# Expert units of 384 or 448 rows, with a transposed second product

## The reference

```
# layer A: every row goes to one expert
expert_idx = argmax(xn @ en.T / tau);  gate_w = softmax(...)[expert_idx]
for e in range(8):
    h = maximum(x[mask] @ w1[e], 0);  out[mask] = gate_w * (h @ w2[e])
# layer B, on layer A's rows: rows with x @ w_skip > 0 alone are computed
e_idx = argmax(x @ w_gate);  gate_w = softmax(...)[e_idx]
out = x + gate_w * (maximum(x @ w1[e], 0) @ w2[e])     # other rows: out = x
```

## Time and profile before

| | us |
|---|---|
| median of 3 runs | 739.09 |
| the profiled execution | 744.15 |
| its span, first to last instruction | 742.4 |
| TensorE matmul busy | 676.3 (91%) |
| VectorE busy | 440.2 (59%) |
| ScalarE busy | 316.8 (43%) |
| GpSimd busy | 170.1 (23%) |
| mean granted TensorE clock | 0.954 |

### The profile page before, as it was taken

How to read it: one execution, slowest core, us unless ns; L and a number is a source line. 1 busy time by engine, 2 the same in 40 slices (tenths; PEclk the granted TensorE clock), 3 DMA queues, 4 the chain that set the end, 5 groups by cost and what they waited for, 6 DMA issues and landing times.

```text
span 742.4 us, 16385 instructions
## 1 busy us (share of the span) xinstructions
PE 676.3 (91%) x5328; PEld 649.5 (87%) x5329; DVE 440.2 (59%) x987; ACT 316.8 (43%) x548; POOL 170.1 (23%) x195
## 2 busy tenths in 40 slices
PE   5999999999879999999899999997699999998992
PEld 4999899998769999989889999997699999998892
DVE  5787978978527455573555655643356564555630
ACT  3565666755215435342534444431253443535520
POOL 4221233252430030321233203123210110111111
PEclk9899999999589999999999999998599999999997
DMA  9688998790145526340701552500266724645400
GB/s 155 86 139 141 172 188 147 98 189 19 64 142 203 174 86 213 119 167 17 254 20 51 206 199 72 167 29 23 80 230 215 253 83 178 231 147 196 140 1 23
DMA packets 142882, 98.65 MB, mean 133 GB/s; under 512 B 106431, under 2 KB 133738, under 8 KB 142816
## 3 DMA queue, kind: packets, MB, share of 16 engines
q1 hardware_dynamic: 135520, 85.14, 44.6%
q0 software_dynamic: 7296, 12.73, 4.9%
HBM read 78.77 MB, written 28.89 MB: 145 GB/s over the span
## 4 chain that ended last, share of the span: by engine, by line
PE 74%; DVE 9%; issue 9%; ACT 3%; DMA 2%; SPq 1%; DVEq 1%; POOL 0%; ACTq 0%; POOLq 0%
PE bank_a L922 6%; PE banks_y L798 6%; PE bank_a L924 6%; PE bank_a L923 6%; PE banks_y L932 5%; PE banks_y L934 5%; PE banks_y L933 5%; PE banks_s L777 3%; DVE w_lo L1313 3%; PE bank_a L853 3%; PE bank_b L934 2%; PE bank_b L932 2%; PE bank_b L933 2%; PE banks_y L790 2%; PE bank_b L922 2%
## 5 line engine op out<-in xcount | busy, mean ns | idle before, releaser
L1313 DVE TENSOR_TENSOR w_lo<-raw_w,w_hi 128x768 fp32r<-128x768 f32 x128 | 116.6, 953 | 8.6 <-DVE kept L1664 3.6
L922 PE MATMUL bank_a<-x_hi,w_hi 128*128 128x384 f32 (+1 forms) x342 | 109.6, 321 | 5.8 <-DVE w_lo L1313 3.1
L924 PE MATMUL bank_a<-x_hi,w_lo 128*128 128x384 f32 (+1 forms) x342 | 106.8, 312 | 0.0
L923 PE MATMUL bank_a<-x_lo,w_hi 128*128 128x384 f32 (+1 forms) x342 | 106.8, 312 | 0.0
L1195 ACT ACTIVATE h_hi<-bank_a 128x384 fp32r<-128x384 f32 (+1 forms) x114 | 50.2, 440 | 122.9 <-PE bank_a L924 122.8
L1063 ACT ACTIVATE w_hi<-raw_w 128x768 fp32r<-128x768 f32 x128 | 99.2, 839 | 0.0
L636 POOL DMA_INDIRECT sorted_rows<-row_send,slot_idx x33 | 36.0, 1090 | 232.2 <-DVE slot_idx L1586 225.5
L1620 DVE SCALAR_TENSOR_TENSOR h_lo<-bank_a,h_hi 128x384 fp32r<-128x384 f32 (+1 forms) x114 | 55.8, 493 | 50.6 <-ACT h_hi L1195 47.8
L932 PE MATMUL banks_y<-w_hi,h_hi 128*128 128x384 f32 x232 | 79.8, 344 | 2.1 <-DVE row_out L1602 1.2
L934 PE MATMUL banks_y<-w_hi,h_lo 128*128 128x384 f32 x232 | 78.1, 337 | 0.0
L933 PE MATMUL banks_y<-w_lo,h_hi 128*128 128x384 f32 x232 | 78.0, 336 | 0.0
(11 more groups left out here) (216 smaller groups left out, 1399.5 us busy)
## 6 DMA issues: line engine op xcount, KB each, us to landing
raw_w<-in_moe_w SPq DMA_DIRECT2D x30, 1536.0 KB, 7.0
sorted_rows<-pad_row SPq DMA_DIRECT2D x16, 388.0 KB
raw_f<-in_f_logit SPq DMA_DIRECT2D x32, 144.0 KB, 4.3
raw_k<-in_k SPq DMA_DIRECT2D x32, 144.0 KB, 4.3
raw_q<-in_q SPq DMA_DIRECT2D x32, 144.0 KB, 4.9
raw_v<-in_v SPq DMA_DIRECT2D x32, 144.0 KB, 3.1
xs<-sorted_rows SPq DMA_DIRECT2D x22, 194.0 KB, 4.3
xs<-sorted_rows SPq DMA_DIRECT2D x10, 388.0 KB, 5.0
```

What stands on the lines that cost most here:

```text
L922: pe.matmul(bank, hi, x_hi[:, kd, cols], start=(kd == 0), stop=False)
L923: pe.matmul(bank, hi, x_lo[:, kd, cols], start=False, stop=False)
L924: ins = pe.matmul(bank, lo, x_hi[:, kd, cols], start=False, stop=(kd == KD - 1))
L1313: dve.tensor_tensor(w_lo[par][:, sl, :], raw_w[:, sl, :], w_hi[par][:, sl, :].bitcast(F32), ALU.subtract).then_inc(w_split_lo, 1)
```

## The change

Layer A gets code of its own. Its plan (`plan_mixed`) counts an expert's rows in blocks of 64 and makes units of 448 rows (`LARGE`) or 384 rows (`SMALL`): up to 6 blocks are one small unit, 7 blocks one large unit, more are large units and at most one small one. The second product is transposed as well: w2 stationary, the unit's hidden values moving, 24 matmuls for each of three blocks of 128 output columns. ScalarE copies its result, `y_t`, and both the logits and the rows are made from it in the next unit: `route_logits` uses `y_t` as it is, `turn_rows` turns it back with 12 transposes, and VectorE scales each tile straight into `row_send`. The next unit's rows are loaded, turned and split within the second product. There are four slots of rows for a unit, the fourth with 64 rows. Layer B keeps the old units; it waits for four slots to be sent, and `row_out` is now the same memory as `row_send`.

```diff
-    REG = N + 2 * P
+    REG = N + 3 * P
+    MIXED_SLOTS = 4
+    SMALL, LARGE = 3 * P, 3 * P + HB
+        y_t = sb("y_t", [P, KD, LARGE])
...
+        def over_mixed(engine, unit):
+            engine.wait_ge(plan_ready[0], 1)
+            with engine.Fori(0, E // 2) as e2:
+                for par in range(2):
...
+                    with engine.If(small > 0):
+                        unit(par, e, u0, SMALL, 0, small)
+                    with engine.If(larges > 0):
+                        with engine.Fori(0, larges) as j:
+                            unit(par, e, u0 + small + j, LARGE, j, small)
...
# SP
+                        sp.wait_ge(f["kept"], u + 1)
+                        load_mixed(size, e * REG + j * LARGE + small * (0 if size == SMALL else SMALL))
+                        def next_expert():
+                            with sp.If(e < E - 1):
+                                pad(within(e + 1, 1, E - 1))
...
+                            wait_split(sp, e, 1)
+                            load_next(0, e, par, load_w1)
+                            wait_split(sp, e, 2)
+                            load_next(0, e, par, load_w2)
...
# TensorE
+                def take_mixed(next_u, s=s):
+                    pe.wait_ge(s["xs_first"], 16 * (next_u + 1))
+                    pe.wait_ge(s["xs_second"], 16 * (next_u + 1))
+                    for kd in range(KD):
+                        for slot in range(SLOTS):
+                            pe.transpose(ps_take[kd][:, slot * P:(slot + 1) * P], xs[0][:, slot, kd * P:(kd + 1) * P], ident[:])
+                        pe.transpose(ps_take[kd][:, SMALL:LARGE], xs_more[:, kd * P:(kd + 1) * P],
+                                     ident[0:HB, 0:HB]).then_inc(s["xt"], 1)
+                def contract_mixed(par, size, kd, kf):
+                    bank = ps_yt[kd][:, 0:size]
+                    hi, lo = (w2_slice(w[par][:], kf)[:, kd * P:(kd + 1) * P] for w in (w_hi, w_lo))
+                    pe.matmul(bank, hi, h_hi[:, kf, 0:size], start=(kf == 0), stop=False)
+                    pe.matmul(bank, hi, h_lo[:, kf, 0:size], start=False, stop=False)
+                    return pe.matmul(bank, lo, h_hi[:, kf, 0:size], start=False, stop=(kf == KF - 1))
+                def unit_mixed(par, e, u, size, j, small, s=s):
+                    wait_split(pe, e, 1)
+                    pe.wait_ge(s["x_lo"], KD * u + KD)
+                    for kf in range(KF):
+                        if kf >= 3:
+                            pe.wait_ge(s["h_lo"], KF * u + kf - 2)
+                        expand_mixed(par, size, kf)
+                        if kf == 0:
+                            route_logits(u)
+                        if kf == 1:
+                            turn_rows(u)
+                        if kf == 4:
+                            rank(g, u + 1, MIXED_SLOTS, ps_rank_u, ps_count_u)
+                    wait_split(pe, e, 2)
+                    pe.wait_ge(s["row"], MIXED_SLOTS * u + 7)
+                    for kd in range(KD):
+                        if kd == 2:
+                            pe.wait_ge(s["y_copied"], KD * u + KD + 1)
+                        for kf in range(KF):
+                            if kd == 0:
+                                pe.wait_ge(s["h_lo"], KF * u + kf + 1)
+                            ins = contract_mixed(par, size, kd, kf)
+                            if kd == 1 and kf == 2:
+                                take_mixed(u + 1)
+                        ins.then_inc(s["y"], 1)
...
+                def route_logits(u, s=s):
+                    pe.wait_ge(s["y_copied"], KD * u + KD)
+                    pe.wait_ge(g["slot"], u + 1)
+                    for slot in range(MIXED_SLOTS):
+                        n = slot_rows(slot)
+                        for kd in range(KD):
+                            ins = pe.matmul(ps_logit_u[0:n, slot, 0:E + 1], y_t[:, kd, slot * P:slot * P + n], gate_w_t[:, kd, :],
...
+                def turn_rows(u, s=s):
+                    pe.wait_ge(s["row"], MIXED_SLOTS * u + 3)
...
+                            ins = pe.transpose(ps_row[slot][0:n, kd * P:(kd + 1) * P], y_t[:, kd, slot * P:slot * P + n], ident[:])
+                        ins.then_inc(s["turned"], 1)
...
# ScalarE, unit_mixed
+                    for kf in range(KF):
+                        act.wait_ge(s["h"], KF * u + kf + 1)
+                        act.activation(h_hi[:, kf, 0:size], ps_h[kf % 3][:, 0:size], ACT.Relu).then_inc(s["h_hi"], 1)
+                        if kf == 4:
+                            softmax(g, u, MIXED_SLOTS)
+                    in_first_mixed(act, size, j, small, lambda: split_four(e + 1, 1 - par, w1_in, 0))
+                    copy_y(size, u, 0)
+                    x_high_mixed(u + 1)
...
+                    in_first_mixed(act, size, j, small, second_weights)
+                    copy_y(size, u, 1)
+                    copy_y(size, u, 2)
...
# VectorE, unit_mixed, behind the low part of each block kf
+                        if kf == 1:
+                            pick_rows(ch, u)
+                        if kf == 3:
+                            rows_to_send((0, 1), u)
+                        if kf == 4:
+                            rows_to_send((2, 3), u)
+                            keep_mixed(ch, size, u)
+                        if kf == 6:
+                            place_rows(ch, u)
+                    in_first_mixed(dve, size, j, small, lambda: split_four(e + 1, 1 - par, 0))
+                    x_low_mixed(u + 1)
...
+                    in_first_mixed(dve, size, j, small, second_weights)
...
+            def rows_to_send(slots, u):
...
+                    dve.wait_ge(s["turned"], MIXED_SLOTS * u + slot + 1)
+                    dve.tensor_scalar(row_send[0:n, slot, 0:DM], ps_row[slot][0:n, :], kept[0:n, slot, 0:1], None,
+                                      ALU.mult).then_inc(s["row"], 1)
...
+            def keep_mixed(ch, size, u):
...
+                dve.wait_ge(s["row"], MIXED_SLOTS * u + 7)
+                ch.link(dve.tensor_copy(kept[:, 0:SLOTS, :], xs[0][:, :, GATE:GATE + 2]))
...
+                dve.tensor_copy(kept[0:HB, SLOTS, :], more).then_inc(s["kept"], 1)
...
# pick_rows
-                ch.link(dve.tensor_reduce(mx, ps_logit_u[:, :, 0:E], AX.X, ALU.max))
+                ch.link(dve.tensor_tensor(scored[:], ps_logit_u[:, :, 0:E + 1],
+                                          gates.rearrange("p (c o) -> p c o", o=1).to_broadcast((P, nt, E + 1)), ALU.mult))
+                ch.link(dve.tensor_reduce(mx, scored[:, :, 0:E], AX.X, ALU.max))
...
# plan_mixed
+                ch.link(dve.tensor_scalar(blocks, counts, float(HB - 1), None, ALU.add))
+                whole(ch, 0, blocks, blocks, 6)
+                ch.link(dve.tensor_scalar(units, blocks, 37.0, None, ALU.mult))
+                whole(ch, 0, larges, units, 8)
...
# after the loop: TensorE, then VectorE
+                    route_logits(last)
+                    turn_rows(last)
+                    rank(g, last + 1, MIXED_SLOTS, ps_rank_u, ps_count_u)
...
+                    keep_warm(bank_a, JUNK_A[1])
...
+                    pick_rows(ch, last)
+                    rows_to_send(range(MIXED_SLOTS), last)
+                    place_rows(ch, last)
+                    plan_pairs(ch)
```

More of the change, by code:

```diff
@@ L265, in in_range @@
         def in_range(value, low, high):
-            return nc.s_assert_within(value, low, high, skip_runtime_bounds_check_because="made so by make_plan")
+            return nc.s_assert_within(value, low, high, skip_runtime_bounds_check_because="made so by the plan")
         def units_of(engine, m, e):
@@ L489, in expert @@
                         with sp.If(e < 1):
[L490 to L495, removed]
+                            for k in range(MIXED_SLOTS):
+                                sp.wait_ge(row_sent[k], 16 * units_before)
+                                settle(sp)
+                            sp.wait_ge(fs[0]["xt"], KD * units_before + KD)
                             settle(sp)
@@ L692, in _ @@
         def _(pe):
-            for count in from_one_pe:
-                pe.sem_inc(count, 1)
             pe.wait_ge(const_ready, 2)
@@ new lines, in count_rows, with whole, finish_plan @@
+                return counts
+            def whole(ch, m, dst, src, shift):
+                ch.link(dve.tensor_copy(plan[m][:, 1, :], src))
+                ch.link(dve.tensor_single_scalar(plan[m][:, 1, :], plan[m][:, 1, :], shift, ALU.arith_shift_right))
+                ch.link(dve.tensor_copy(dst, plan[m][:, 1, :]))
+            def finish_plan(ch, m, units, sizes):
+                before, first = plan_f[:, 3, :], plan_f[:, 2, :]
+                ch.link(dve.memset(before, 0.0))
+                ch.link(dve.tensor_tensor_scan(first, units, before, 0.0, ALU.add, ALU.add))
+                ch.link(dve.tensor_tensor(before, first, units, ALU.subtract))
```

(10 more changed lines are left out.)

379 lines of the change are left out of this document (222 added, 157 removed).

## The result

The changed kernel takes 801.69 us (median of 4 runs, 799.07 to 804.96) against 739.48 us for the kernel before on the same chip: a ratio of 1.084 [1.080, 1.089]. It is 8.4% slower; the forecast was 714.1 us and faster. The profiled execution took 799.07 us, with a span of 797.3.

A forecast was written before the change was run, and what follows sets the result against it. TensorE, 91% busy, was taken to bound the kernel. Loop -30.0, losses +1.5 and serial stretch +3.5 gave -25.0 us: profiled execution 744.15 to 719.2, median 739.09 to 714.1, range 706 to 727.

The forecast's parts named there:

- the lead-in's 1.2 and 2.9: Before layer A's first product: 1.2 us for extra plan_mixed steps, about 2.9 us for the first take and its split.
- the serial stretch: From layer A's last product to layer B's first turn: 3.5 us longer than the 21.6 before.
- Unit boundaries: Between layer A's units on TensorE: the earlier 1.13 us "issue" wait disappears, so no gap was counted.
- Rival 2: The gap at layer A's unit boundaries stays, 1.1 us a unit, 8.8 us more, 723 us; chance 0.07.
- Rival 6: The clock falls in layer A's first unit, half clock for 6 us costing 3 us, 717 us; chance 0.08.
- Routing at 5.0 us a unit: TensorE's turns, logit products, places and changes between kinds in each layer A unit: 5.0 us in all.
- The width of 448: Layer A matmuls of 448 columns on TensorE: 0.204 us each, against 0.1768 for 384 columns.
- rival 3: Layer A's 448-column matmuls cost less, 0.190 us each, 6 us less in all, 708 us; chance 0.08.
- rival 5: Layer A's plan makes other than 8 units, say one more of 30.5 us, 744 us; chance 0.02.
- The row loop: Keep, load, take in each layer A unit: next rows land in time, with slack of about 1 us.
- Rival 1: Every layer A unit stalls on late rows or VectorE's order, 1.5 us each, 724.6 us; chance 0.15.
- rival 4: Layer A's rows land in 9 us or more, each unit waiting 3.2 us beyond slack, 741 to 751 us; chance 0.05.

The follow-up runs named there:

- experiment 2: Changed kernel with only TensorE's layer A loop head placed at slot 0 of a 256-instruction fetch block: 746.92 us, ratio 1.005 to the kernel before.
- 5: Changed kernel with TensorE's layer A loop head at position 144 of a 256-instruction fetch block: 793.72 us, ratio 1.073 to the kernel before.
- 3: Kernel before, plus 40 never-executed blank matmuls in each half of TensorE's layer A loop: 807.87 us, ratio 1.090 to the kernel before.
- 1: Changed kernel with units of 448 rows alone in layer A, one body in each half: 775.3 us, ratio 1.046 to the kernel before.
- 7: Kernel of 1 with its small logit products and turns spread between the first product's pieces: 765.77 us, ratio 1.035 to the kernel before.
- 4: Kernel of experiment 2 with its small logit products and turns spread between the first product's pieces: 730.99 us, ratio 0.987 to the kernel before.
- experiment 8: Kernel of experiment 4 with 80 more blank products on TensorE ahead of the first take: 729.28 us, ratio 0.984 to the kernel before.
- 9: Kernel of experiment 8 with a branch prefetch hint on TensorE in units of 384 rows: 729.23 us, ratio 0.984 to the kernel before.

## Why the prediction was wrong, step by step

The profiled execution was to take 719.2 us and took 799.07, 79.9 more. By stage: the loop from its first to its last product took 341.1 us (219.55 to 560.6) where the forecast has 255.7 and 1.5 of losses, +83.9; its first product came 4.7 us early (219.55, where 220.1 with the lead-in's 1.2 and 2.9 gives 224.2); the serial stretch to layer B's first turn +0.2; from there on +0.5.

- **The step that failed** is "Unit boundaries": "After, the unit also ends in 24 matmuls without a wait, so I count no gap." The term stood at nothing, and the six gaps are 44.7 us. I took "issue" for the echo of a wait ahead of a branch, looked only at the instruction next to the branch, and never asked how long the code behind the branch is. The change puts two long bodies in each half, and the loop outgrows what TensorE keeps. Experiments 2 and 5 show it by position, 3 by length alone. That reading of the 1.1 us itself was not refuted: where the loop stays, a unit that ends in 24 matmuls has no gap behind it (experiment 2 behind the first pass, 1 and 7). Rival 2 had a gap at every unit, at 8.8 us in all and for another reason.
- **The clock** failed with it: 33.1 us lost. Of these 28.0 stand within 16 us behind the six gaps, where a clump of logits stands too, so that this trace alone doesn't part the two; the unit at 434, with its clump and no gap, has no dip. Rival 6 had the clock fall in the first unit at 3 us; the first unit does dip (0.50 from 225 to 230) and loses 5.1. The part that the clumped logits cost was in neither the sum nor a rival. I had costed the clump at 2.32 us of its own time, which is right (2.4), and not what it does to the matmuls behind it (experiments 2 and 4, 1 and 7).
- **Routing at 5.0 us a unit** was too low. A unit of 384 without losses takes 31.6 us (take to take, 428.46 to 460.09 in experiment 8), one of 448 35.7, so 6.1 and 6.3 beside the products. The take is the reason; in experiment 8:

```profile
428.46 0.49 PE L998 MATMUL bank_a<-ident,xs 128*128 128x128 f32 x3
...
430.45 0.44 PE L1019 MATMUL bank_b<-h_hi,w_hi 128*128 128x384 f32 x1
```

  That is 1.99 us for 12 turns, where I had 0.96. I took the price of the turns of outgoing rows (0.24 for three) for those of incoming ones; a row for the right kind, six turns with a duration of 0.87 us, stood in the earlier trace rows; from start to start six take 0.71 us (278.15 to 278.86). Over eight units it is some 9 us, and with 44.7 and 33.1 it makes 87 for the loop's 83.9 beyond the forecast: the parts close to within 3 us, the clock's sum being rough.
- **The width of 448** held. Three starts in the second half of a large unit of the changed kernel:

```profile
367.22 0.36 PE L1007 MATMUL bank_a<-x_hi,w_hi 128*128 128x448 f32 x1
...
367.83 0.36 PE L1007 MATMUL bank_a<-x_hi,w_hi 128*128 128x448 f32 x1
```

  0.61 us for three, 0.203 each, against 0.204: rival 3 (0.190) falls. The plan has the 8 units (5 and 3), so rival 5 falls.
- **The row loop** held. The next rows landed in 3.0 us (388 KB) and 4.3 us (582 KB), not 5.0 and 5.5, and no unit of the changed kernel waited for them inside the second product. Rival 1, the likeliest of the rivals, and rival 4 play no part. Rival 4's price was also worked out wrong: with the load free to start at 15.7 and the take at 22.5, a landing of 9 us is 2.2 us late and not 3.2, and one of 10.5 is 3.7 late and not 4.6.
- **The serial stretch** held: from the last product's end to layer B's first turn 25.3 us (560.6 to 585.87) against 21.6, +3.7 for the +3.5 forecast. From there to the end 211.4 us against 210.9.

With both faults mended and nothing else changed, the kernel is 1.3% faster than before (experiment 4), and 1.6% with more blank matmuls in front (8 and 9); the loop is 272 to 284 us in the profiled executions. The change can pay, at half of the 25 us that were forecast.

## What to carry to other kernels

Before a change that adds a body to a loop, count the instructions of that loop on each engine, and look in the DMA queues for instruction fetches in the steady part of the loop. No entry in the queue of the engine that bounds the loop (q8 here; q14 had some even before) means that its code stays, and that this can be lost. "Issue" gaps at jumps together with such fetches are code; move the loop's head, share a body, or take code out before anything else is tuned. A releaser that the profile names is not proof of a wait: ask whether the transfer named is the one that the instruction needs (experiment 3). Small products cost the clock here in a clump of twelve and did not in threes between large ones.

## What was not expected of the hardware

- The same instructions with the loop at another position differ by 7% (1.005 and 1.073), and 40 products in each half that never run cost 9%.
- A wait for code was 2 to 10 us in the changed kernel, and the clock's fall after it cost nearly as much again: 44.7 us of gaps and 33.1 of lost clock.
- The clock can fall while TensorE is busy 5.00 of 5.00 us, after 2.4 us of products of 9 columns in one clump; the same products in threes, between large matmuls, left it at 1.00 for 170 us.
- Open: why executions of one kernel differ in mean clock (0.946 to 0.966 in the six of experiment 9), with 11 us between them; and the gap that a hint did not take away.
